# Moving the fourth batch of sorted rows ahead of the row softmax in the tail of a recurrence and two-MoE kernel

## The reference, cut to what matters

```python
attn_out = _attn_ref(**attn_kwargs)          # a linear recurrence over 768 steps, 4 x 8 heads of 48
x = attn_out.transpose(0, 2, 1, 3).reshape(B * S, H * D)      # 3072 rows of 384
x = _moe_ref(x=x, **moe_kwargs)              # rows that pass a gate go through one of 8 experts
return _moe2_ref(x=x, **moe2_kwargs)         # soft MoE, below

def _moe2_ref(x, phi, w1, w2):               # phi: 384 x 32 slots
    logits = x @ phi
    d = np.exp(logits - logits.max(0, keepdims=True))
    d /= d.sum(0, keepdims=True) + 1e-09     # softmax over the rows: "dispatch"
    slot_input = (d.T @ x).reshape(E, S_per_e, D)
    for e in range(E):
        h = np.maximum(slot_input[e] @ w1[e], 0.0)
        slot_out[e] = h @ w2[e]
    c = np.exp(logits - logits.max(1, keepdims=True))
    c /= c.sum(1, keepdims=True) + 1e-09     # softmax over the slots: "combine"
    return c @ slot_out.reshape(n_slots, D)
```

## Time and profile before

| | us |
|---|---|
| median of 3 runs | 381.19 |
| lowest and highest | 380.25, 381.48 |
| span of the profiled execution, first to last instruction | 387.5 |

### The profile page before, as it was taken

How to read it: one execution, slowest core, us unless ns; L and a number is a source line. 1 busy time by engine, 2 the same in 40 slices (tenths; PEclk the granted TensorE clock), 3 DMA queues, 4 the chain that set the end, 5 groups by cost and what they waited for, 6 DMA issues and landing times.

```text
span 387.5 us, 14814 instructions
## 1 busy us (share of the span) xinstructions
PE 354.1 (91%) x5880; PEld 269.6 (70%) x5880; DVE 281.8 (73%) x564; ACT 221.0 (57%) x681; POOL 115.0 (30%) x179
## 2 busy tenths in 40 slices
PE   6699999999999999889999999999999999679990
PEld 6487777877777788656777777777777777345360
DVE  7999999999999634786676767777677776430371
ACT  3777888778887755134656556565555664200060
POOL 3543322343223340254222233332221224540000
PEclk9989999999999999989999999999999999689996
DMA  8987656766568995013193799495858779759438
GB/s 310 415 305 265 241 198 216 257 258 248 197 205 286 424 402 205 3 23 111 29 393 128 300 323 393 178 361 193 325 211 321 263 259 396 281 170 327 167 152 336
DMA packets 31300, 97.58 MB, mean 252 GB/s; under 512 B 4062, under 2 KB 14410, under 8 KB 29722
## 3 DMA queue, kind: packets, MB, share of 16 engines
q1 hardware_dynamic: 29466, 93.81, 65.2%
q0 software_dynamic: 1792, 3.17, 2.7%
HBM read 85.53 MB, written 11.45 MB: 250 GB/s over the span
## 4 chain that ended last, share of the span: by engine, by line
PE 56%; DVE 5%; another core or an unknown queue 3%; issue 1%; POOL 1%; ACT 1%; DVEq 0%; ACTq 0%
PE a_bank L772 19%; PE y_bank L781 18%; PE y_bank L928 3%; PE a_bank L944 3%; PE a_bank L637 2%; DVE x_all L1550 2%; PE sums_bank L705 1%; PE a_bank L832 1%; PE y_bank L598 1%; PE y_bank L593 1%; PE ktok_bank L645 1%; PE sums_bank L645 1%; PE y_bank L605 1%; PE y_bank L740 0%
## 5 line engine op out<-in xcount | busy, mean ns | idle before, releaser
L781 PE MATMUL y_bank<-w_sb,work 128*32 128x192 f32 x1664 | 78.5, 326 | 0.5 <-ACT work L1131 0.5
L772 PE MATMUL a_bank<-w_sb,work 128*32 128x256 f32 x1248 | 77.9, 382 | 0.1
L781 PEld LDWEIGHTS y_bank<-w_sb,work 128*32 128x32 f32 x1664 | 64.9, 110 | 8.8 <-DVE work L1396 1.1
L1586 POOL TENSOR_SCALAR_AFFINE_SELECT a_sb<-a_sb 128x512 f32<-128x512 f32 x48 | 44.2, 932 | 86.7 <-ACT a_sb L1016 86.7
L772 PEld LDWEIGHTS a_bank<-w_sb,work 128*32 128x32 f32 x1248 | 42.4, 109 | 25.6 <-issue 13.0
L1026 ACT ACTIVATE bonus_v<-v_sb,bonus 128x48 f32<-128x48 f32 x192 | 45.0, 321 | 14.0 <-DVE x_all L1260 13.9
L1104 ACT ACTIVATE work<-work 32x96 f32<-32x96 f32 x108 | 30.4, 281 | 39.3 <-PE a_bank L772 37.0
L1440 DVE TENSOR_TENSOR ys<-work 32x192 f32<-32x192 f32 x104 | 37.0, 355 | 9.9 <-ACT work L1131 9.2
L1396 DVE STREAM_TRANSPOSE work<-hid 128x256 f32<-128x256 f32 x53 | 23.6, 446 | 26.2 <-PE y_bank L781 22.9
L572 PE MATMUL a_bank<-r_in,k_in 64*128 64x128 f32 x384 | 31.0, 295 | 0.1
L572 PEld LDWEIGHTS a_bank<-r_in,k_in 64*128 64x128 f32 x384 | 24.7, 193 | 6.3 <-issue 5.7
(11 more groups left out here) (314 smaller groups left out, 582.6 us busy)
## 6 DMA issues: line engine op xcount, KB each, us to landing
w_sb<-in_moe_w SPq DMA_DIRECT2D x20, 1536.0 KB, 11.7
wrk_sb<-in_wrk SPq DMA_DIRECT2D x16, 768.0 KB, 7.0
e_sb<-in_moe_w SPq DMA_DIRECT2D x8, 1536.0 KB, 11.0
wrk_sb<-in_wrk SPq DMA_DIRECT2D x15, 780.0 KB
v_sb<-in_vt SPq DMA_DIRECT2D x16, 288.0 KB, 2.9
tokens<-x_all SPq DMA_DIRECT2D x4, 1152.0 KB, 21.7
out<-x_all SPq DMA_DIRECT2D x12, 384.0 KB, 3.9
x_all<-in_moe_w SPq DMA_DIRECT2D x2, 1536.0 KB
```

Of the source, the lines that this page charges most:

```text
L772: last = nc.tensor.matmul(out[SUB * g:SUB * (g + 1), 0:FB], x[:, kk, :], w1_sb[j][:, kk, FB * g:FB * (g + 1)], start=(kk == 0), stop=(kk = ...
L781: last = nc.tensor.matmul(bank[4][SUB * g:SUB * (g + 1), 0:YW], h_t[:, SUB * k:SUB * (k + 1)], w2_sb[j][:, k, d:d + YW], start=(b == 0), s ...
L1586: nc.gpsimd.affine_select(out=x, in_=x, compare_op=ALU.is_gt, fill=0.0, base=0, pattern=[[0, 2], [0, 2], [1, C]], channel_multiplier=-1).t ...
```

## The change

PE turns the fourth batch right behind the scores of the third; the combine turns and the first dispatch turn come behind the loop. DVE and ACT follow with their shifts and exponentials. No operation is added. `idle_products(2, spare_place)`, which is four records, is dropped. On POOL two waits change places.

```diff
@@ tensor
             early_scores(1)
-            pe.wait_ge(y_parts_ready, ends[E] + 1)
-            combs_turn(0)
             early_scores(2)
-            combs_turn(1)
-            pe.wait_ge(weigh_ready, 3)
-            pe.wait_ge(logit_t_ready, 3)
-            turn(weigh_t, weigh_turned, 0, 2, bank[5][:, 2 * P:4 * P])
             with pe.Fori(0, rest) as t:
...
                 slot_scores(x_t4[1], bank[6], stage_turned)
+            pe.wait_ge(weigh_ready, 3)
+            turn(weigh_t, weigh_turned, 0, 2, bank[5][:, 2 * P:4 * P])
+            pe.wait_ge(y_parts_ready, ends[E] + 1)
+            combs_turn(0)
             pe.wait_ge(disp_ready, 3)
             dispatch(0, B1, 0, B1, x_sorted, bank[0])
-            combs_turn(2)
             pe.wait_ge(part_top_ready, 1)
             nc.tensor.transpose(bank[2][0:1, 0:P], part_top[:, :], ident[:, :]).then_inc(tops_turned, 1)
-            idle_products(2, spare_place)
+            combs_turn(1)
             pe.wait_ge(weigh_ready, 4)
...
             turn(weigh_t, weigh_turned, 4, XQ, bank[6])
+            combs_turn(2)
             dispatch(3 * BATCH, LAST_GROUPS, B1, MAX_GROUPS, x_sorted, bank[1])
@@ scalar
-            weigh(2, 0, 2, 2)
-            comb_exps(0)
             with act.Fori(0, rest) as t:
...
-            comb_exps(1)
+            weigh(2, 0, 2, 2)
             copy_disp(3, 0, 2 * BATCH, bank[5][:, 2 * P:4 * P])
             weigh(3, 2, 4, 3)
+            weigh(3, 4, XQ, 4)
             copy_disp(4, 2 * BATCH, 4 * BATCH, bank[5])
-            weigh(3, 4, XQ, 4)
+            comb_exps(0)
             act.wait_ge(less_top_ready, 1)
...
             copy_disp(5, 4 * BATCH, TILES, bank[6])
+            comb_exps(1)
             comb_exps(2)
@@ vector
-            shift_combs(0)
             logits_of(2)
-            shift_combs(1)
             with dve.Fori(0, rest) as t:
...
             dve.sem_inc(less_part_ready, 1)
-            shift_combs(2)
+            shift_combs(0)
             dve.wait_ge(tops_turned, 1)
...
                             -1.0, None, ALU.mult).then_inc(top_row_ready, 1)
+            shift_combs(1)
             V.memset(flat_t[:, 0:E * DK * NS], 0.0).then_inc(slots_clear, 1)
...
             V.tensor_copy(less_top[:, :], bank[3][:, 0:1]).then_inc(less_top_ready, 1)
+            shift_combs(2)
             dve.wait_ge(rescale_ready, 1)
@@ gpsimd
+            wait(ld_rows_in, 16 * groups + 32)
             wait(x2_done, groups + 1)
-            wait(ld_rows_in, 16 * groups + 32)
             pool.sem_inc(x2_done, 3 * BATCH)
```

## The result

| | before | changed |
|---|---|---|
| median, us | 379.98 | 381.74 |
| lowest to highest | 379.11 to 383.48 | 380.33 to 383.36 |
| runs | 20 | 20 |

The ratio of changed to before is 1.0039, with a 95% interval of 1.0021 to 1.0056. The whole interval lies above 1, so the change made the kernel slower, by about 1.5 us, where 1.0 us of gain was forecast. Repeated on another chip it gave 1.0057 [1.0031, 1.0082]. The profiled execution of the changed kernel took 382.77 us with a span of 381.0, and this execution is 1.0 us above the median. The difference of some 1.8 us between time and span is there in every execution for which both are recorded. So the span of before in the earlier trace rows belongs to an execution of some 389.3 us, 9 above the median.

The account below looks back on a forecast made before the run. PE's chain from the fourth batch's blocks to the experts' first product was taken as the bound. 1.4 gained, 1.0 lost and 0.6 returned gave 1.0 us: 381.19 to 380.2 us, range 378.2 to 382.8.

Parts of the forecast that it names:

- Items 1 and 2: Fourth batch on PE and DVE: blocks start 1.55 us earlier, copies end sooner and fourth scores start 1.4 us earlier.
- item 1: PE before the fourth batch: third scores start at 323.45 instead of 323.76, blocks at about 324.15, 1.55 us earlier.
- Items 3 to 6: Dispatch up to the fold: exposed turn and copy lose 1.0 us, a shift, turn and idle products return 0.6.
- Item 6: DVE before the fold: two added shifts, 1.24 us, just fit 1.3 us of cover; otherwise 0.3 us is lost.
- Item 7: ACT, POOL, SP: exponentials move into ACT's idle time, stage copies do not hold PE, expert 4's load lands tenths early.
- The gaps: Idle of 3.45 us before the fourth logits and 2.75 after the fold, taken as mostly the profiled execution's alone.
- The rival built on them: Gaps before the fourth logits are real in every run and the change shrinks them: 378.4 us, chance 0.14.
- The rival of the puts: Later exponentials delay POOL's puts, so the tables' sum comes late: 1.6 us slower, 382.8 us, chance 0.21.
- so the margin is about one microsecond: Tables' sum: read back about 0.7 us late, against a sum ending 1.5 us before the product needing it.
- with both gaps closed PE's chain is 6.2 us earlier behind the puts: PE against POOL's puts: closing both gaps, plus 1.0 from the change, makes the tables' read back due at 352.6.
- 3.4 us of waits fall away: POOL's waits before the fifth and ninth put, 1.88 and 1.55 us, vanish if puts land within their round.

Follow-up runs that it names:

- e10: The kernel before, unedited, profiled again on a chip without gaps: 380.82 us, ratio 1.0008.
- e15: The kernel before without the third batch's four puts, on a chip without gaps: 379.87 us, ratio 0.999.
- e16: The changed kernel without the third batch's four puts, on the same chip as e15: 379.49 us, ratio 0.997.
- e5: The changed kernel, unedited, run again on a chip without gaps: 382.24 us, ratio 1.0057 to the kernel before.
- e3: The changed kernel without the third batch's four puts, on a chip with gaps: 382.68 us, ratio 0.988 to the kernel before.
- e12: The kernel before without the third batch's four puts, on another chip with gaps: 385.02 us, ratio 0.9953.
- e8: The changed kernel without the third batch's four puts, on a chip without gaps: 378.93 us, ratio 0.9961 to the kernel before.
- e4: The changed kernel with the first combine batch's turn, shift and exponential back ahead of the loop, with gaps: 386.99 us, ratio 0.9957 to the kernel before.
- e13: e4 plus POOL counting each table as it lands and SP reading them one by one, with gaps: 387.33 us, ratio 0.9992 to the kernel before.
- e9: The changed kernel with the second and third batches' puts sent to eight unread tables, so no round waits: 381.05 us, ratio 1.0017 to the kernel before.
- e18: The changed kernel, unedited, run again on a chip without gaps: 381.75 us, ratio 1.0032 to the kernel before.
- e1: The kernel before, unedited, profiled again on a chip with gaps: 387.06 us, ratio 1.0004.
- e14: The kernel before with tables counted and read back one by one, on a chip with gaps: 385.77 us, ratio 0.9966.
- e2: The kernel before with only ACT's first two combine exponentials moved later, on a chip with gaps: 385.77 us, ratio 0.9959.

## Why the prediction was wrong, point by point

**Items 1 and 2 (blocks and fourth scores 1.5 and 1.4 us earlier).** Right. Scores to scores, third to fourth, it is 3.05 us now (326.28 - 323.23) and was 4.21, with the third scores themselves 0.3 earlier behind the first (3.02 us against 3.30), as item 1 had them.

**Items 3 to 6 (what is given back on PE, ACT and DVE).** Right: first dispatch 0.36 us after an idle for ACT's copy, 0.34 us of cover left on DVE. Item 6 put the cover without gaps at 1.3 us before the two shifts, and `e10` has 1.40. The sum of 1.0 us measured 0.86 between `e15` and `e16`.

**Item 7 (ACT, POOL, SP).** PE's blocks were not held by the stage copies. The load of expert 4 was in time in the changed kernel's first trace and 0.34 us late in `e5`. That the moved exponentials cost nothing on ACT was right; what they do to POOL was left to the rival, and there the error lies.

**The gaps.** They were taken as closed in the usual execution. On three of the five chips of the experiments that was right, and on two it was not. The rival built on them, that the change shrinks them, stays open: the changed kernel itself did not run on a chip with gaps. For it speaks `e3`, the changed kernel with fewer puts: on a chip with gaps it took 382.68 us, all its runs between 382.51 and 383.09, and its trace has no gap before the fourth logits (DVE's timeline):

```profile
328.02 0.29 DVE L1480 TENSOR_TENSOR free_rows<-ktok_bank,free_rows 128x128 f32 x1 [1.30 <-PE ktok_bank L840]
```

The kernel before with the same edit, `e12`, took 385.02 and has the gap. They ran on different chips. In `e3` PE still needs 41.79 us from its first scores to the end of the experts, where `e8` needs 38.30, and `e4` and `e13`, close to the changed kernel, have gaps of 3.40 and 4.76 us later on (DVE line 1519). So `e3` is a hint and no more.

**The rival of the puts.** This is the case that came true. Its price of 1.6 us slower is about what was measured (1.5), and its time of 382.8 compares with 381.74. That the price comes so close is partly luck: it was worked out from 3.4 us of waits more, and the size of what is late was far off. The step that failed is the one on which its chance rested: "so the margin is about one microsecond", from which the puts would come only 0.7 us late. (The margin itself was read a little too wide: PE goes into line 698 at 369.12, 1.4 us and not 1.5 behind the sum's end at 367.75; 369.25 is DVE's line 1540.) Two terms of it were off, both in the same direction.

First, "with both gaps closed PE's chain is 6.2 us earlier behind the puts", so that the read back "is due at 352.6". A gap took more than its own length: behind the first the granted clock stood at 0.50, behind the second at 0.52 (346 to 348 us), and in `e10` it is 1.00 in all these stretches. By line 928 the kernel before is 9.1 us earlier without gaps, where 6.2 was reckoned (it ends at 349.22 in `e10` and at 358.36 in the profiled execution before). In the changed kernel line 926 ends at 347.68, and line 521, 1.34 behind line 519 as in `e15`, was due at 349.0, 3.6 us before 352.6.

Second, "3.4 us of waits fall away", and a last landing in "some 2.4 us". The waits before the fifth and the ninth put measured 1.73 and 2.58 us, 4.3 together, and the read back followed the last put by 4.46 (353.04 to 357.50). From first put to last it is 21.5 us now and was 22.4 (348.57 - 326.21), 22.7 in `e10`: the sequence moved almost as it was. The Trainium skill (DMA: Bandwidth & Descriptors, "Anatomy of one DMA") gives a small transfer some 2.0 us; the changed kernel's trace disagrees, with 3.2 to 6.8 us and a median of 5.2, and only the last put of `e9`, on nearly idle DMA engines, comes close with 2.2.

So the last table could be read 8.5 us after it was due (357.50 against 349.0), where 0.7 was reckoned. Of this PE pays only 2.82 us. The two adds start with tables 1 to 3, whose read back is 5.4 us late. It lands sooner than an early one: from line 519 to DVE's first addition it is 5.45 us here (353.15 to 358.60) and 6.62 in `e15` (349.53 to 356.15), which takes off 1.2. The experts' second layer keeps PE busy until 358.5, which covers about as much again. The account without gaps: 2.82 of new wait, less the 0.86 gained, less the 0.5 that the puts cost the kernel before already (a difference whose interval just holds zero), is 1.5 us slower, against 1.5 between the first medians. The 2.82 comes from an execution 1.0 us above its median; in `e18` the same account gives 1.2 (2.54 of wait) where its runs gave 1.65, and in `e5` 1.5 (2.27 of wait and 0.3 gained, since its stretch on PE is 38.92 us) where its runs gave 2.0. So it holds to about half a microsecond. The chance of 0.21 was too low because the argument assumed that waits behind a landing fall away when the puts leave later, with nothing in the profile that said so: the DMA engines' share is 1.06 beside the fifth put still.

## What to carry to other kernels

When a step is moved behind another to free the bound engine, follow its products all the way to where they are needed again, here through four scatters a batch, a landing and a read back, and put the margin against the time of an undisturbed execution, with the clock of that execution. A wait for a DMA does not go away because the DMA starts later; price it as it stands unless the profile shows that the DMA engines are free at its new place. And where a consumer waits for several transfers at once, let it take each as it lands. Here the change gave +0.4%, with the first combine batch back ahead of the loop +0.1% (not clear of zero), and with the tables read one by one as well -0.4%.

## What the runs showed of the hardware that was not expected

**Late updates from PE, on some chips only.** The kernel before took 387.6 and 386.6 us on two chips, and 380.2, 380.2, 380.33 and 380.1 in the groups on the others. The traces on the two chips have "remote" gaps behind PE's products, before the fourth logits in `e1`, `e12` and `e14` (3.57 to 4.35 us of idle), at DVE's line 1519 in `e4` and `e13`, and at neither place in `e2` and `e3`. The timeline of DVE and two windows of `e12` show one, where the scores had ended at 329.0 by the profile:

```profile
332.38 0.29 DVE L1484 TENSOR_TENSOR free_rows<-ktok_bank,free_rows 128x128 f32 x1 [4.35 <-remote]
```

```profile
330.00:332.00 2.00, 0.58 (x5) 0.14 (x1) 0.00 (x0) 0.00 (x0) 1.02 (x2) 1.00 1.07 387
334.00:336.00 2.00, 2.00 (x12) 1.49 (x15) 1.32 (x5) 0.77 (x2) 1.61 (x2) 0.50 0.85 305
```

PE is busy 0.58 us of the two ahead of the update, and then works at granted clock 0.50, 1.2 GHz. In `e10`, without the gap, the window from 334 has clock 1.00. What makes the updates late is open, and so is whether the products or only the update end late.

**A put of 128 short rows landed in 2 to 3 us on quiet DMA engines and in up to 7 beside weight loads.** The fifth put of the changed kernel took 6.8 us, with the DMA engines' share at 1.06 from 338 to 344. The eleventh, issued at 348.43, took 3.2 with a mean share of 0.37 until it landed, the twelfth of `e5` 3.0 at 0.17, and the thirteenth of `e9`, issued at 350.13, 2.2 at 0.11. The median of the ten that the changed kernel's trace has is 5.2 us. These are a few puts, and the cause of the difference was not tested by itself. Windows of the changed kernel:

```profile
338.00:344.00 6.00, 6.00 (x120) 3.60 (x116) 1.52 (x3) 0.38 (x1) 3.93 (x4) 1.00 1.06 385
...
348.43:351.63 3.20, 3.20 (x42) 1.21 (x38) 0.00 (x0) 0.34 (x2) 1.96 (x2) 1.00 0.37 118
```

and of `e9`:

```profile
350.13:352.33 2.20, 2.20 (x36) 0.85 (x32) 0.00 (x0) 0.01 (x1) 1.00 (x1) 1.00 0.11 35
```
